# Retention attention and two expert layers on one core: order of the first loads, four sums on GpSimd, one more tile, the order of x's sums, and where h lies

## The chip, the cores and the metric

One NeuronCore of one Trainium2 chip runs the whole program in one launch. The metric is the time of the device in microseconds. The kernel before took 1574.39 us in the median of three runs (1574.02 to 1576.73).

## The reference

Inputs are float32. Three stages follow each other on the same 1536 tokens (batch 2, sequence 768) of 512 features.

```python
# 1. retention attention, 8 heads of 64, decay gamma_h = 1 - 2**(-5-h)
state = gamma * state + outer(k[t], v[t]);  y[t] = q[t] @ state / 8      # for t in 768
x = y.transpose(0, 2, 1, 3).reshape(1536, 512)
# 2. eight experts, all used for every token, Sinkhorn gates
P = exp(x @ w_gate - max);  eight times: normalise rows, then columns, times N/E
x = sum_e P[:, e:e+1] * (relu(x @ w1[e]) @ w2[e])                        # w1 512x1024, w2 1024x512
# 3. four experts with gates that come as an input (rows normalised)
out = sum_e p[:, e:e+1] * (relu(x @ w1[e]) @ w2[e])
```

## The kernel before

**Attention.** The sequence is cut into six chunks of 128 positions; with two batches that makes twelve steps s, c = s // 2 the chunk and b = s % 2 the batch. TensorE computes in step order: score(s+1) (line 893), then attend(s): the product of state and raised q (line 913, not in chunk 0), the sum of k and v into the state (line 925, not in the last chunk), and scores by v (line 931). attend(s) writes one of three PSUM banks in turn, so attend(s) from s = 3 on waits until chunk (s-3)//2 has been read out of its bank: by `x_summed` and `x_lo0`, and for a bank of batch 1 by `x_lo1` as well. VectorE masks scores (line 557). GpSimd multiplies k by a decay (line 312) and q by a rise (line 325), and waits for `y_done` before each rise. Each engine works strictly in the order in which its instructions are written.

**x.** Each float32 operand of the expert layers is held as a high and a low fp32r part. x is also needed in four sums of its quarters (names T1 to T4, tile `x_sum`), because the first product of an expert is done by seven products on half-size blocks, in place of eight. For chunk n ScalarE runs `x_high0` (line 370, batch 0), `x_high1` (line 381 copies quarter B12 into the place of T3 in `x_sum`, line 382 the high part of B22) and `sums_high` (line 386). VectorE runs `x_sums` (line 563, four subtractions; the fourth writes T3 over the copy of B12), `x_low0`, `x_low1` and `sums_low` (all line 592); for the last two chunks `sums_low` is GpSimd's (line 330). As B12 is copied into `x_sum`, `x_high1(n)` waits until `sums_low(n-1)` has read `x_sum`.

**Experts.** Each of the 12 experts is done in two halves of its 1024 hidden features, k = 0 to 23, and each of these over two blocks p of 384 positions of both batches. up(k, p) is 84 products of 384 columns (lines 1010, 1012, 1014): stationary w1_hi or w1_lo, moving x_hi or x_lo. down(k, p) is 72 products of 512 columns (lines 1031 to 1033): stationary h_hi or h_lo, moving w2_hi or w2_lo. The hidden values h are made by ScalarE and VectorE. w1 comes by one DMA of 1 MB into `w_raw`; `w1_sums` (lines 602 to 608, VectorE) makes three sums of its quarters and leaves a fourth in place; `split_w1_high` (ScalarE, lines 416 to 423) and `split_w1_low` (VectorE, line 592, parts 0 to 3) split them. w2 comes into the same `w_raw` once all four parts are done. For k = 0 all this is written into the last steps of attention: `w1_sums(0)` after VectorE's step 9, part 0 of the high halves after ScalarE's step 10, and VectorE's low parts 0 and 1 in step 11, parts 2 and 3 after `x_sums(5)`. Of up(0, 0), product 0 (12 matmuls) needs w1's low part 0; product 1 waits until ScalarE has copied product 0 out (line 467), and ScalarE has `sums_high(5)` ahead of that copy. After up(0, 0) come 40 matmuls with `wg_parts` for the gates (lines 959, 961), 384 columns, stationary `wg_parts`, moving x_hi or x_lo.

**Loads.** SP issues, in order: k_t and q_t of step 0, the mask, v and k of step 0, then q/k, v and k of step 1, and so on; from step 4 on it waits for `y_done` of step s-4 before the loads of step s. Expert w1(0) is issued after the loads of step 8. ScalarE's queue issues kdecay, rise, step, ident, w_gate and the gates of layer 3; the last two arrive in runs of 32 and 16 bytes.

**Places.** Tiles are placed in SBUF one behind the other, each from a multiple of 32 bytes. x_hi, x_lo, w1_hi, w1_lo, w2_hi and w2_lo begin at the same place modulo 512 bytes. Then come small tiles and `place`, and then, overlaid, attention's tiles or h_hi, h_lo, ups and acc: these begin 192 bytes behind that place modulo 512. `wg_parts` begins 320 bytes behind it.

Of the kernel before, what the change touches and what calls it, by code (L numbers as in the profile page):

```python
# [9 lines left out]
ALU = mybir.AluOpType  # L10
# [4 lines left out]
P = 128  # L15
BATCH, HEADS, SEQ, HD = 2, 8, 768, 64
DM = HEADS * HD
DC = DM // P
NTOK = BATCH * SEQ
NSUB = NTOK // P  # L20
# [9 lines left out]
BANK = 512  # L30
SINKHORN = 8
EPS = 1e-9
WARM = 10
GAMMA = [1.0 - 2.0 ** (-5.0 - h) for h in range(HEADS)]


# [24 lines left out]
def retention_moe_moe_kernel(nc, q_t, k_t, k, v, moe_w_gate, moe_w1, moe_w2, moe2_probs, moe2_w1, moe2_w2,  # L61
# [3 lines left out]
    with ctx:  # L65
        def sb(name, shape, dt=F32, scope=None):
            return (scope or ctx).enter_context(nc.sbuf_tensor(name, shape, dt))
# [16 lines left out]
        w2_hi = sb("w2_hi", [P, UC, DM], F32R)  # L84
        w2_lo = sb("w2_lo", [P, UC, DM], F32R)
        x_sum = sb("x_sum", [P, 4 * 2, P])
        ident = sb("ident", [P, P])
        act_warm = sb("act_warm", [P, 2])
        gate1 = sb("gate1", [P, NSUB, E1])
# [8 lines left out]
        step = sb("step", [P, DC])  # L98


        sb("place", [P, 48])

# [127 lines left out]
        @block.sync  # L232
        def _(sp):
            def load_qk(c, b):
                r = c % 2
                sp.dma_start(kt_in[r][b][:, :, :], k_t[b, c].rearrange("p (c t) -> p c t", c=DC)).then_inc(qk_in[r][b], 16)
                sp.dma_start(qt_in[r][b][:, :, :], q_t[b, c].rearrange("p (c t) -> p c t", c=DC)).then_inc(qk_in[r][b], 16)

            def load_k(c, b):
                r = c % 2  # L240
                sp.dma_start(k_in[r][b][:, :, :], k[b, c].rearrange("t (h d) -> t h d", h=HEADS)).then_inc(
                    k_in_s[r][b], 16)

            def load_v(c, b):
                r = c % 2
                sp.dma_start(v_in[r][b][:, :, :], v[b, c].rearrange("t (h d) -> t h d", h=HEADS)).then_inc(
                    v_in_s[r][b], 16)

            def load_w1(w, e, s):
                src = w[bass.ds(e, 1), :, s * UF:(s + 1) * UF].rearrange("a (c p) f -> p (a c) f", p=P)  # L250
                sp.dma_start(w1_raw, src).then_inc(w1_in, 16)

            def load_w2(w, e, s):
                src = w[bass.ds(e, 1), s * UF:(s + 1) * UF, :].rearrange("a (c p) n -> p (a c) n", p=P)
                sp.dma_start(w2_raw, src).then_inc(w2_in, 16)

            load_qk(0, 0)
            sp.dma_start(mask[:, :, :, :], c_mask.rearrange("p (r c j) -> p r c j", r=2, c=DC)).then_inc(mask_in, 16)
            load_v(0, 0)
            load_k(0, 0)  # L260
            load_qk(0, 1)
            load_v(0, 1)
            load_k(0, 1)
            for s in range(2, STEPS):
                c, b = s // BATCH, s % BATCH
                if c > 1:

                    sp.wait_ge(y_done, s - 4 + 1)
                load_qk(c, b)
                load_v(c, b)  # L270
                if c < CH - 1:
                    load_k(c, b)
                if s == 8:
                    load_w1(moe_w1, 0, 0)

            def weights(w1, w2, e, k, last=False):
                sp.wait_ge(w1_ready, 4 * k + 4)
                load_w2(w2, e, 0)
                sp.wait_ge(w2_ready, 2 * k + 2)
                load_w1(w1, e, 1)  # L280
                sp.wait_ge(w1_ready, 4 * k + 8)
                load_w2(w2, e, 1)
                if not last:
                    sp.wait_ge(w2_ready, 2 * k + 4)

            with sp.Fori(0, E1 - 1) as e:
                weights(moe_w1, moe_w2, e, 2 * e)
                load_w1(moe_w1, e + 1, 0)
            weights(moe_w1, moe_w2, E1 - 1, 2 * (E1 - 1))
            load_w1(moe2_w1, 0, 0)  # L290
            with sp.Fori(0, E2 - 1) as e:
                weights(moe2_w1, moe2_w2, e, 2 * e + 2 * E1)
                load_w1(moe2_w1, e + 1, 0)
            weights(moe2_w1, moe2_w2, E2 - 1, 2 * (E1 + E2 - 1), last=True)

            last = 2 * (E1 + E2) - 1
            stores = [(0, 3), (0, 6), (1, 1), (1, 2), (1, 3), (1, 4), (1, 5), (1, 6)]
            for p, n in stores:
                sp.wait_ge(acc_written, downs_before(last, p) + n)
                rows = [row_of(p, u) for u in (range(n - CPB, n) if p == 0 else [n - 1])]  # L300
                sp.dma_start(out_d[:, rows[0]:rows[-1] + 1, :], acc[:, rows[0]:rows[-1] + 1, :]).then_inc(stored, 16)
            sp.wait_ge(stored, 16 * len(stores))
# [3 lines left out]
        def _(pool):  # L306
# [29 lines left out]
            decay_k(0)  # L336
            decay_k(1)
            nc.gpsimd.memset(wg_parts[:, :, :].bitcast(F32), 0.0).then_inc(wg_zeroed, 1)
            for s in range(BATCH, STEPS):
                raise_q(s)  # L340
                if s < STEPS - BATCH:
                    decay_k(s)
            for n in range(CH - 2, CH):
                sums_low(n)

# [11 lines left out]
        def _(act):  # L357
            act.dma_start(kdecay[:, :, :], c_kdecay.rearrange("p (c h) -> p c h", c=CH - 1)).then_inc(kdecay_in, 16)
            act.dma_start(rise[1][:, :, :], c_rise.rearrange("p (c t) -> p c t", c=DC)).then_inc(rise_in, 16)
            act.dma_start(step[:, :], c_step).then_inc(rise_in, 16)  # L360
            act.dma_start(ident[:, :], c_ident).then_inc(ident_in, 16)
            act.dma_start(wg_raw[:, :, :], moe_w_gate.rearrange("(c p) e -> p c e", p=P)).then_inc(wg_in, 16)
            act.dma_start(gate2[:, :, :], moe2_probs.rearrange("(i p) e -> p i e", p=P)).then_inc(gate2_in, 16)

            def x_high0(n, from_acc=False):
                if from_acc:
# [6 lines left out]
            def x_high1(n, from_acc=False):  # L373
                if from_acc:
                    act.wait_ge(x2_transposed, BATCH * (n - CH) + 2)
                else:
                    act.wait_ge(y_done, BATCH * n + 2)
                if n > 0:

                    act.wait_ge(x_lot, n)  # L380
                nc.scalar.copy(x_sum[:, 4:6, :], x_bank(n, 1)[:, 0:2, :]).then_inc(x_b12, 1)
                nc.scalar.copy(x_hi[:, X_B22, :, x_at(n)], x_bank(n, 1)[:, 2:4, :]).then_inc(x_hi1, 1)

            def sums_high(n):
# [42 lines left out]
            nc.scalar.copy(act_warm[:, 1:2], act_warm[:, 0:1])  # L427
            for s in range(STEPS):
                c, b = s // BATCH, s % BATCH
                if b == 1:  # L430
                    x_high0(c)
                elif c > 0:
                    x_high1(c - 1)
                if c < CH - 1:
                    state_out(s, b)
                if b == 0 and c > 0:
                    sums_high(c - 1)
                if b == 0 and 2 <= c + 2 < CH:
                    rise_out(c + 2)
                if s == STEPS - 2:  # L440
                    split_w1_high(0, 0, first=True)
                if s == STEPS - 1:
                    split_w1_high(0, 1)
            act.wait_ge(wg_in, 16)
            act.wait_ge(wg_zeroed, 1)
            nc.scalar.copy(wg_parts[:, :, 0:E1], wg_raw[:, :, :]).then_inc(wg_hi_ready, 1)
# [95 lines left out]
        def _(dve):  # L542
# [18 lines left out]
            def x_sums(n):  # L561
                def sub(o, a, b):
                    return nc.vector.tensor_tensor(o, a, b, ALU.subtract)  # L563

                t1, t2, t3, t4 = [x_sum[:, 2 * i:2 * i + 2, :] for i in range(4)]
                y0, y1 = x_bank(n, 0), x_bank(n, 1)


                dve.wait_ge(x_b12, n + 1)

                dve.wait_ge(x_hi1, n + 1)
                then_wait(sub(t1, t3, y0[:, 0:2, :]))
                then_wait(sub(t2, y1[:, 2:4, :], t1))
                sub(t4, y0[:, 2:4, :], t2)
                sub(t3, y1[:, 2:4, :], t3).then_inc(x_summed, 1)

            def x_low0(n):
                dve.wait_ge(x_hi0, n + 1)
# [12 lines left out]
            def low(out, raw, high):  # L591
                return nc.vector.tensor_tensor(out, raw, high.bitcast(F32), ALU.subtract)  # L592

            def w1_sums(k, first=False):
                a11, a21 = w1_raw[:, 0:2, 0:2 * P], w1_raw[:, 0:2, 2 * P:4 * P]
                a12, a22 = w1_raw[:, 2:4, 0:2 * P], w1_raw[:, 2:4, 2 * P:4 * P]
                s2, s3, s4 = w1_sum[:, 0, :, :], w1_sum[:, 1, :, :], w1_sum[:, 2, :, :]
                dve.wait_ge(w1_in, 16 * k + 16)
                if not first:

                    dve.wait_ge(w1_ready, 4 * k)
                nc.vector.tensor_tensor(s3, a11, a21, ALU.subtract).then_inc(w1_summed, 1)
                dve.wait_ge(w1_summed, 4 * k + 1)
                nc.vector.tensor_tensor(a21, a21, a22, ALU.add).then_inc(w1_summed, 1)
# [40 lines left out]
            mask_scores(0)  # L645
            for s in range(STEPS):
                c, b = s // BATCH, s % BATCH
                if s < STEPS - 1:
                    mask_scores(s + 1)
                if b == 1:  # L650
                    x_low0(c)
                    if 0 < c < CH - 1:
                        sums_low(c - 1)
                elif c > 0:
                    x_sums(c - 1)
                    x_low1(c - 1)
# [476 lines left out]
```

## Time and profile before

| | |
|---|---|
| median of three runs | 1574.39 us |
| the profiled execution's own time | 1574.22 us |
| its span, first to last instruction | 1572.4 us |
| mean granted TensorE clock | 0.997 |
| TensorE busy | 1553.9 us, 99% of the span |
| VectorE, ScalarE, GpSimd busy | 884.4, 445.8, 51.4 us |

What lies around the span in the profiled execution is 1.8 us. Matmuls are pipelined: one is recorded as longer than the distance from its start to the next start, and that distance, the pitch, is what counts. Line numbers are those of the kernel before.

### The profile page before, as it was taken

The numbers are of one execution on the slowest core, as the hardware profiler recorded it, in microseconds if no ns is written. First come the engines' busy times: TensorE is split into PE (matmuls) and PEld (weight loads), VectorE is DVE, ScalarE is ACT, GpSimd is POOL, SyncE is SP. The second block draws the span as 40 slices with busy tenths as digits, with TensorE's granted clock in tenths as the row PEclk, the third lists the DMA queues.
The fourth block names the chain that finished last, engine by engine and source line by source line (L and its number), as shares of the span: only waits on it lengthen the run. The fifth ranks groups of instructions, "written<-read, shape, count | busy, mean of one in ns | idle before, by whom it ended". The sixth has DMA issues, their size and how long they took to land.

```text
span 1572.4 us, 21277 instructions
## 1 busy us (share of the span) xinstructions
PE 1553.9 (99%) x8232; PEld 1404.6 (89%) x8232; DVE 884.4 (56%) x1437; ACT 445.8 (28%) x860; POOL 51.4 (3%) x42
## 2 busy tenths in 40 slices
PE   8899999999999999999999999999999999999999
PEld 7798899889989988998899889988998899889988
DVE  6846766455555465464455554667545546545553
ACT  4422223213313222232133222333322223213321
POOL 5200000000000000000000000012000000000000
PEclk9899999999999999999999999999999999999999
DMA  9201001011010010110110100101001011011011
GB/s 325 86 3 54 26 28 54 0 54 54 1 53 27 27 53 2 51 53 0 53 38 15 53 27 28 54 0 55 27 28 54 10 45 54 0 53 53 1 42 67
DMA packets 36491, 67.28 MB, mean 43 GB/s; under 512 B 4048, under 2 KB 4176, under 8 KB 36432
## 3 DMA queue, kind: packets, MB, share of 16 engines
q1 hardware_dynamic: 33776, 66.07, 12.1%
q8 instruction: 41, 0.67, 0.2%
q10 hardware_dynamic: 2656, 0.39, 0.2%
q14 instruction: 18, 0.15, 0.0%
HBM read 63.31 MB, written 3.15 MB: 42 GB/s over the span
## 4 chain that ended last, share of the span: by engine, by line
PE 96%; DVE 2%; issue 1%; ACT 1%; DMA 1%; SPq 0%; DVEq 0%; ACTq 0%
PE bank L1032 17%; PE bank L1031 17%; PE bank L1033 17%; PE bank L1010 15%; PE bank L1014 15%; PE bank L1012 15%; DVE x_sum L563 1%; DMA qt_in<-in_q_t 1%; DVE x_lo L592 0%; PE bank L978 0%; DVE scores L557 0%; ACT rise L405 0%; PE bank L961 0%; PE bank L959 0%; ACT x_hi L370 0%
## 5 line engine op out<-in xcount | busy, mean ns | idle before, releaser
L1032 PE MATMUL bank<-w_lo,h_hi 128*128 128x512 f32 x1152 | 453.7, 394 | 0.0
L1010 PE MATMUL bank<-x_hi,w_hi 128*128 128x384 f32 x1344 | 450.6, 335 | 3.0 <-DVE w_lo L592 1.3
L1031 PE MATMUL bank<-w_hi,h_hi 128*128 128x512 f32 x1152 | 451.9, 392 | 0.0
L1014 PE MATMUL bank<-x_hi,w_lo 128*128 128x384 f32 x1344 | 450.1, 335 | 0.0
L1012 PE MATMUL bank<-x_lo,w_hi 128*128 128x384 f32 x1344 | 449.8, 335 | 0.0
L1033 PE MATMUL bank<-w_hi,h_lo 128*128 128x512 f32 x1152 | 447.3, 388 | 0.0
L756 DVE SCALAR_TENSOR_TENSOR acc<-bank,gate,acc 128x512 f32<-128x512 f32 x252 | 189.2, 751 | 379.7 <-PE bank L1033 379.7
L467 ACT COPY ups<-bank 128x384 f32<-128x384 f32 x288 | 138.7, 482 | 911.6 <-PE bank L1014 911.6
L709 DVE TENSOR_TENSOR ups<-bank,ups 128x384 f32<-128x384 f32 x288 | 155.4, 554 | 191.2 <-ACT ups L467 169.5
L1033 PEld LDWEIGHTS bank<-w_hi,h_lo 128*128 128x128 f32 x1152 | 216.3, 188 | 48.3
L1031 PEld LDWEIGHTS bank<-w_hi,h_hi 128*128 128x128 f32 x1152 | 216.2, 188 | 48.2
L1010 PEld LDWEIGHTS bank<-x_hi,w_hi 128*128 128x128 f32 x1344 | 252.8, 188 | 6.1 <-issue 2.3
L1012 PEld LDWEIGHTS bank<-x_lo,w_hi 128*128 128x128 f32 x1344 | 252.8, 188 | 1.8
L1032 PEld LDWEIGHTS bank<-w_lo,h_hi 128*128 128x128 f32 x1152 | 216.6, 188 | 41.3
L1014 PEld LDWEIGHTS bank<-x_hi,w_lo 128*128 128x128 f32 x1344 | 252.7, 188 | 0.0
L470 ACT ACTIVATE h_hi<-ups 128x384 fp32r<-128x384 f32 x288 | 148.0, 524 | 134.3 <-DVE ups L709 134.3
L714 DVE SCALAR_TENSOR_TENSOR h_lo<-ups,h_hi 128x384 fp32r<-128x384 f32 x288 | 156.2, 557 | 12.3
L592 DVE TENSOR_TENSOR w_lo<-w_raw,w_hi 128x1024 fp32r<-128x1024 f32 x96 | 114.8, 1217 | 0.0
L714 DVE SCALAR_TENSOR_TENSOR h_lo<-bank,h_hi 128x384 fp32r<-128x384 f32 x96 | 53.6, 558 | 2.2
L470 ACT ACTIVATE h_hi<-bank 128x384 fp32r<-128x384 f32 x96 | 47.3, 493 | 12.7
L330 POOL TENSOR_TENSOR x_lo<-x_sum,x_hi 128x1024 fp32r<-128x1024 f32 x8 | 20.1, 2514 | 903.8 <-ACT x_hi L386 903.8
L592 DVE TENSOR_TENSOR w_lo<-w_sum,w_hi 128x1024 fp32r<-128x1024 f32 (+1 forms) x48 | 46.3, 965 | 0.0
(76 smaller groups left out, 498.2 us busy)
## 6 DMA issues: line engine op xcount, KB each, us to landing
w_raw<-in_moe_w SPq DMA_DIRECT2D x48, 1024.0 KB, 5.1
kt_in<-in_k_t SPq DMA_DIRECT2D x12, 256.0 KB, 4.4
qt_in<-in_q_t SPq DMA_DIRECT2D x12, 256.0 KB, 5.9
v_in<-in_v SPq DMA_DIRECT2D x12, 256.0 KB, 6.0
k_in<-in_k SPq DMA_DIRECT2D x10, 256.0 KB, 6.4
out<-acc SPq DMA_DIRECT2D x2, 768.0 KB, 4.5
out<-acc SPq DMA_DIRECT2D x6, 256.0 KB, 2.0
mask<-in_c_mask SPq DMA_DIRECT2D x1, 512.0 KB, 5.7
```

The source lines that it names most:

```text
L467: nc.scalar.copy(ups[:, half, slot, :], up_psum(ON_X, half)).then_inc(copied, 1)
L470: nc.scalar.activation(h_hi[:, f, b, :], src, ACT.Relu).then_inc(h_hi_ready, 1)
L592: return nc.vector.tensor_tensor(out, raw, high.bitcast(F32), ALU.subtract)
L709: nc.vector.tensor_tensor(ups[:, half, slot, :], up_psum(kind, half), ups[:, half, slot, :], ALU.add).then_inc(summed, 1)
L714: nc.vector.scalar_tensor_tensor(h_lo[:, f, b, :], src, 0.0, h_hi[:, f, b, :].bitcast(F32), ALU.max, ALU.subtract).then_inc(h_ready, 1)
L756: nc.vector.scalar_tensor_tensor(a, y, gate[:, i, bass.ds(col, 1)], a, ALU.mult, ALU.add).then_inc(acc_written, 1)
L1010: nc.tensor.matmul(o, w1_hi[:, w, kc, fs], x_hi[:, x, kc, at], start=start and kc == 0, stop=False, skip_group_check=True)
L1012: nc.tensor.matmul(o, w1_hi[:, w, kc, fs], x_lo[:, x, kc, at], start=False, stop=False, skip_group_check=True)
L1014: last = nc.tensor.matmul(o, w1_lo[:, w, kc, fs], x_hi[:, x, kc, at], start=False, stop=kc == 1, skip_group_check=True)
L1031: nc.tensor.matmul(o, h_hi[:, f, b, rows], w2_hi[:, f, :], start=(n == 0), stop=False)
L1032: nc.tensor.matmul(o, h_hi[:, f, b, rows], w2_lo[:, f, :], start=False, stop=False)
L1033: last = nc.tensor.matmul(o, h_lo[:, f, b, rows], w2_hi[:, f, :], start=False, stop=(n == UC - 1))
```

## The change

- SP's loads come in the order of use: q and k_t of a step, then k and v of the step before. So v(0), k(0) stand behind q/k of step 1, and from step 4 on k and v of step s-1 stand behind the wait of step s. w1(0) moves from behind step 8's loads to before step 11's wait. ident and the gates of layer 3 move from ScalarE's queue to the end of SP's attention loads. w_gate and the gates of layer 3 are laid out in the partition order by the host, so that each partition is one run.
- The first w1 sums go from VectorE to GpSimd: two of them before the rise of q of step 11, two behind it.
- B12 has its own tile `b12` (1024 bytes). `x_high1(n)` then waits for `x_summed` of chunk n-1, and `x_sums(n)` waits for `x_lot`.
- VectorE's `x_sums(c-1)` is ahead of `mask_scores(s+1)` in even steps. At the end the order is low part 0, `x_low0(5)`, low parts 1, 2, 3, `x_sums(5)`, `x_low1(5)`. ScalarE's high part 0 of w1 is after `sums_high(4)` in program order as before, and its second half is behind `x_high0(5)`.
- `place` grows from 192 to 512 bytes. With b12's 1024 that moves attention's tiles and h_hi, h_lo, ups and acc by 1344 bytes: their offset modulo 512 to w2 and x goes from 192 to 0, that of `wg_parts` from 320 to 128.
- TensorE's warm-up is 8 matmuls instead of 10.

```diff
-WARM = 10
+WARM = 8
+        b12 = sb("b12", [P, 2, P])
-        sb("place", [P, 48])
+        sb("place", [P, 128])
@@ sync
+            def load_kv(c, b):
+                if c < CH - 1:
+                    load_k(c, b)
+                load_v(c, b)
             load_qk(0, 0)
...
-            load_v(0, 0)
-            load_k(0, 0)
-            load_qk(0, 1)
-            load_v(0, 1)
-            load_k(0, 1)
-            for s in range(2, STEPS):
+            for s in range(1, STEPS):
+                if s == STEPS - 1:
+                    load_w1(moe_w1, 0, 0)
                 if c > 1:
                     sp.wait_ge(y_done, s - 4 + 1)
                 load_qk(c, b)
-                load_v(c, b)
-                if c < CH - 1:
-                    load_k(c, b)
-                if s == 8:
-                    load_w1(moe_w1, 0, 0)
+                load_kv((s - 1) // BATCH, (s - 1) % BATCH)
+            load_kv(CH - 1, 1)
+            sp.dma_start(ident[:, :], c_ident).then_inc(ident_in, 16)
+            sp.dma_start(gate2[:, :, :], moe2_probs.rearrange("p (i e) -> p i e", e=E2)).then_inc(gate2_in, 16)
@@ gpsimd
+            def first_w1_sums():
+                pool.wait_ge(w1_in, 16)
+                nc.gpsimd.tensor_tensor(s3, a11, a21, ALU.subtract).then_inc(w1_summed, 1)
+                pool.wait_ge(w1_summed, 1)
+                nc.gpsimd.tensor_tensor(a21, a21, a22, ALU.add).then_inc(w1_summed, 1)
+                raise_q(STEPS - 1)
+                pool.wait_ge(w1_summed, 2)
+                nc.gpsimd.tensor_tensor(s2, a21, a11, ALU.subtract).then_inc(w1_summed, 1)
+                pool.wait_ge(w1_summed, 3)
+                nc.gpsimd.tensor_tensor(s4, a12, s2, ALU.subtract).then_inc(w1_summed, 1)
@@ scalar
-                    act.wait_ge(x_lot, n)
-                nc.scalar.copy(x_sum[:, 4:6, :], x_bank(n, 1)[:, 0:2, :]).then_inc(x_b12, 1)
+                    act.wait_ge(x_summed, n)
+                nc.scalar.copy(b12[:, :, :], x_bank(n, 1)[:, 0:2, :]).then_inc(x_b12, 1)
+                if s == STEPS - 1:
+                    split_w1_high(0, 0, first=True)
                 if b == 1:
                     x_high0(c)
...
-                if s == STEPS - 2:
-                    split_w1_high(0, 0, first=True)
-                if s == STEPS - 1:
-                    split_w1_high(0, 1)
+            split_w1_high(0, 1)
@@ vector
+                if n > 0:
+                    dve.wait_ge(x_lot, n)
                 dve.wait_ge(x_b12, n + 1)
...
-                then_wait(sub(t1, t3, y0[:, 0:2, :]))
+                then_wait(sub(t1, b12[:, :, :], y0[:, 0:2, :]))
...
-                sub(t3, y1[:, 2:4, :], t3).then_inc(x_summed, 1)
+                sub(t3, y1[:, 2:4, :], b12[:, :, :]).then_inc(x_summed, 1)
...
+                if b == 0 and c > 0:
+                    x_sums(c - 1)
                 if s < STEPS - 1:
                     mask_scores(s + 1)
-                if b == 1:
+                if b == 0 and c > 0:
+                    x_low1(c - 1)
+                elif b == 1 and c < CH - 1:
                     x_low0(c)
-                    if 0 < c < CH - 1:
+                    if c > 0:
                         sums_low(c - 1)
-                elif c > 0:
-                    x_sums(c - 1)
-                    x_low1(c - 1)
-                if s == STEPS - 3:
-                    w1_sums(0, first=True)
-                if s == STEPS - 1:
-                    split_w1_low(0, 0)
-                    split_w1_low(0, 1)
-            x_sums(CH - 1)
+            split_w1_low(0, 0)
+            x_low0(CH - 1)
+            split_w1_low(0, 1)
             split_w1_low(0, 2)
             split_w1_low(0, 3)
+            x_sums(CH - 1)
             x_low1(CH - 1)
```

## Rows read from the trace of the kernel before

**Rows 1.** The page, busy time of each engine, share of the span, instructions.
```profile
PE 1553.9 (99%) x8232; PEld 1404.6 (89%) x8232; DVE 884.4 (56%) x1437; ACT 445.8 (28%) x860; POOL 51.4 (3%) x42
```

**Rows 2.** Busy time by stretch, then granted clock (1.00 is 2.4 GHz), DMA share, GB/s.
```profile
51.20:53.60 2.40, 0.08 (x2) 0.00 (x0) 2.33 (x5) 0.00 (x0) 0.00 (x0) 0.99 0.00 0
53.60:55.60 2.00, 0.00 (x1) 0.01 (x1) 1.93 (x6) 0.03 (x1) 0.00 (x0) 0.50 0.00 0
...
60.90:63.80 2.90, 2.89 (x9) 2.90 (x10) 2.83 (x6) 0.42 (x2) 0.00 (x0) 0.50 0.00 0
...
70.00:1570.00 1500.00, 1498.15 (x7550) 1354.80 (x7548) 835.88 (x1356) 414.10 (x789) 19.23 (x15) 1.00 0.10 35
```

**Rows 3.** Timeline of TensorE in an expert layer: start, us, instruction.
```profile
707.17 0.39 PE L1031 MATMUL bank<-w_hi,h_hi 128*128 128x512 f32 x1
...
723.65 0.33 PE L1010 MATMUL bank<-x_hi,w_hi 128*128 128x384 f32 x1
...
738.23 0.39 PE L1031 MATMUL bank<-w_hi,h_hi 128*128 128x512 f32 x1
```

**Rows 4.** Timeline of TensorE around the 40 matmuls of the gates.
```profile
77.73 0.34 PE L959 MATMUL bank<-x_hi,wg_parts 128*128 128x384 f32 x1
...
84.79 0.39 PE L1031 MATMUL bank<-w_hi,h_hi 128*128 128x512 f32 x1
```

**Rows 5.** Timeline of TensorE in attention.
```profile
10.53 1.16 PE L893 MATMUL bank<-qt_in,kt_in 64*128 64x128 f32 x16 [2.83 <-DMA qt_in<-in_q_t]
...
13.55 1.16 PE L893 MATMUL bank<-qt_in,kt_in 64*128 64x128 f32 x16 [0.38 <-DMA qt_in<-in_q_t]
...
16.61 1.16 PE L893 MATMUL bank<-qt_in,kt_in 64*128 64x128 f32 x16 [0.41 <-DMA qt_in<-in_q_t]
...
20.29 1.16 PE L893 MATMUL bank<-qt_in,kt_in 64*128 64x128 f32 x16
...
37.41 1.16 PE L913 MATMUL bank<-q_up,state 128*128 128x128 f32 x8 [0.60 <-DVE x_sum L563]
...
48.00 1.16 PE L893 MATMUL bank<-qt_in,kt_in 64*128 64x128 f32 x16
...
55.60 2.08 PE L913 MATMUL bank<-q_up,state 128*128 128x128 f32 x8 [4.32 <-DVE x_sum L563]
...
60.91 0.69 PE L1010 MATMUL bank<-x_hi,w_hi 128*128 128x384 f32 x1 [1.32 <-DVE w_lo L592]
...
65.17 0.41 PE L1010 MATMUL bank<-x_hi,w_hi 128*128 128x384 f32 x1 [0.60 <-ACT ups L467]
```

**Rows 6.** Timeline of VectorE in attention and at its end.
```profile
40.86 1.74 DVE L592 TENSOR_TENSOR x_lo<-x_sum,x_hi 128x1024 fp32r<-128x1024 f32 x1
42.52 1.27 DVE L557 TENSOR_TENSOR scores<-bank,mask 128x512 f32<-128x512 f32 x2
...
48.83 1.76 DVE L602 TENSOR_TENSOR w_sum<-w_raw 128x512 f32<-128x512 f32 x1
...
59.64 1.22 DVE L592 TENSOR_TENSOR w_lo<-w_raw,w_hi 128x1024 fp32r<-128x1024 f32 x1
...
61.91 0.41 DVE L563 TENSOR_TENSOR x_sum<-x_sum,bank 128x256 f32<-128x256 f32 x1
...
63.48 0.68 DVE L592 TENSOR_TENSOR w_lo<-w_sum,w_hi 128x512 fp32r<-128x512 f32 x1
```

**Rows 7.** Timeline of ScalarE at the end of attention.
```profile
58.42 0.58 ACT L370 CAST x_hi<-bank 128x512 fp32r<-128x512 f32 x1
...
63.60 1.05 ACT L386 CAST x_hi<-x_sum 128x1024 fp32r<-128x1024 f32 x1 [2.48 <-DVE x_sum L563]
```

**Rows 8.** Timeline of GpSimd.
```profile
43.91 1.27 POOL L325 TENSOR_TENSOR q_up<-qt_in,rise 128x512 f32<-128x512 f32 x1 [0.41 <-PE bank L931]
48.26 1.78 POOL L325 TENSOR_TENSOR q_up<-qt_in,rise 128x512 f32<-128x512 f32 x1 [3.08 <-PE bank L931]
```

**Rows 9.** The page, DMA issues: size, median us to landing.
```profile
w_raw<-in_moe_w SPq DMA_DIRECT2D x48, 1024.0 KB, 5.1
```

More of the change, by code:

```diff
@@ L338, in _ @@
             nc.gpsimd.memset(wg_parts[:, :, :].bitcast(F32), 0.0).then_inc(wg_zeroed, 1)
-            for s in range(BATCH, STEPS):
+            def first_w1_sums():
+                a11, a21 = w1_raw[:, 0:2, 0:2 * P], w1_raw[:, 0:2, 2 * P:4 * P]
+                a12, a22 = w1_raw[:, 2:4, 0:2 * P], w1_raw[:, 2:4, 2 * P:4 * P]
+                s2, s3, s4 = w1_sum[:, 0, :, :], w1_sum[:, 1, :, :], w1_sum[:, 2, :, :]
+                pool.wait_ge(w1_in, 16)
[7 more added lines that the diff above has]
+                nc.gpsimd.tensor_tensor(s4, a12, s2, ALU.subtract).then_inc(w1_summed, 1)
+            for s in range(BATCH, STEPS - 1):
                 raise_q(s)
@@ L342, in _ @@
                     decay_k(s)
+            first_w1_sums()
             for n in range(CH - 2, CH):
@@ L360, in _ @@
             act.dma_start(step[:, :], c_step).then_inc(rise_in, 16)
-            act.dma_start(ident[:, :], c_ident).then_inc(ident_in, 16)
-            act.dma_start(wg_raw[:, :, :], moe_w_gate.rearrange("(c p) e -> p c e", p=P)).then_inc(wg_in, 16)
-            act.dma_start(gate2[:, :, :], moe2_probs.rearrange("(i p) e -> p i e", p=P)).then_inc(gate2_in, 16)
+            act.dma_start(wg_raw[:, :, :], moe_w_gate.rearrange("p (c e) -> p c e", e=E1)).then_inc(wg_in, 16)
             def x_high0(n, from_acc=False):
@@ L592, in low, with w1_sums @@
                 return nc.vector.tensor_tensor(out, raw, high.bitcast(F32), ALU.subtract)
-            def w1_sums(k, first=False):
+            def w1_sums(k):
                 a11, a21 = w1_raw[:, 0:2, 0:2 * P], w1_raw[:, 0:2, 2 * P:4 * P]
@@ L598, in w1_sums @@
                 dve.wait_ge(w1_in, 16 * k + 16)
-                if not first:
-                    dve.wait_ge(w1_ready, 4 * k)
+                dve.wait_ge(w1_ready, 4 * k)
                 nc.vector.tensor_tensor(s3, a11, a21, ALU.subtract).then_inc(w1_summed, 1)
@@ L1123 @@
     laid["k"], laid["v"] = _chunks_by_position(inputs["k"]), _chunks_by_position(inputs["v"])
+    laid["moe_w_gate"] = inputs["moe_w_gate"].reshape(DC, P, E1).transpose(1, 0, 2).reshape(P, DC * E1)
+    laid["moe2_domain_probs"] = inputs["moe2_domain_probs"].reshape(NSUB, P, E2).transpose(1, 0, 2).reshape(P, NSUB * E2)
     arrays, args = {}, []
```

## The prediction

> **What bounds it now.** I read the busy times first: TensorE is busy for 99% of the span, the next engine for 56% [rows 1]. From 70 to 1570 us it lacks 1.85 us of 1500, at full clock [rows 2]. So in the expert layers only the pitch of its matmuls counts, and nothing that VectorE, ScalarE or a DMA saves there. Before 66 us it is otherwise. The timeline of TensorE, with what ended each idle time, shows three kinds of loss: scores that wait for q's load (2.83, 0.38, 0.41 us), state products that wait for `x_sums` (0.60 us, three times, once per chunk; then 4.32 us), and the first expert's products behind low parts of w1 and a copy of `ups` [rows 5]. The first expert product starts at 60.91 and the second product block at 65.17; from there TensorE runs without a gap. The last state product's 4.32 us have a simple source: VectorE is in order, and it does four w1 sums from 48.83 on, the first 1.76 us, before it masks and gets to `x_sums(4)` [rows 6]. In the same stretch the granted clock is at 0.50, that is 1.2 GHz, from 53.6, some 2.4 us after TensorE went idle, to 63.8 [rows 2].
>
> I go by two sums: when does the second product block start (65.17 before), and what is the pitch of the rest.
>
> **Start of attention.** Scores 1, 2 and 3 start at 10.53, 13.55, 16.61 as their q lands [rows 5]: 3.04 us for each MB, 0.76 us for a load of 256 KB. In the new order v and k of one step (two loads) no longer stand ahead of each q, so q(3) is 1.5 us earlier, 15.1. Against it: k(0) now lands after q(1), at 10.53 - 1.5 + 0.76 = 9.8; its decay takes at most the 1.27 us of a rise of the same size [rows 8], the attend then some 1.6 us (a step without state, 3.06 less 0.41 idle less 1.1 for the scores), and k(1) is 3.0 us later: 12.8 + 1.3 + 1.6 = 15.7. That would leave 0.9. For it: 2048 runs of 16 and 32 bytes, and ident, leave the queues; each load should pass faster, by how much no row says. Bounds 0.9 and 2.4, I take 1.7. From step 4 on k and v stand behind a wait, but TensorE wants them over 2 us later than q of the next step, and a step of 1 MB takes 3.0 us of DMA against 3.68 us of TensorE [rows 5]; hidden. Two warm-up matmuls less: nothing, as score(1) waits for a load.
>
> **The pace of attention.** A step without a stall takes 3.68 us (16.61 to 20.29). From 20.29 to 48.00 are seven steps, 27.71 us, so 1.95 are stalls [rows 5]. They come from a ring: `x_sums`, `sums_high`, rise, `x_high0`, `x_low0`, `sums_low` 1.74 us, mask 1.27 us, `x_sums` [rows 6]; ScalarE's copy of B12 sits in it too, behind `sums_low`. With b12 the copy starts as soon as attend is done, and with `x_sums` ahead of the mask it ends 1.3 us earlier, which is more than 0.60. What is next is TensorE itself. The moved mask is late by 1.65 us, but its scores are wanted only 3 us later. VectorE's own work per chunk is about 6.7 us (two pairs of masks 2.5, `x_sums` 1.65, lows 0.6 + 0.35 + 1.7) of 7.36: little air, so 0 to 1.95, I take 1.95. Score(11) then starts at 48.00 - 1.7 - 1.95 = 44.35.
>
> **The end of attention**, in order. GpSimd: rise(10) ends at about 42; w1 is issued near 35.5 and takes 5.1 us [rows 9] to 8 behind the loads ahead, so at 41 to 43; two sums of 1.27 us (1.78 where VectorE reads SBUF at the same time [rows 8]), then rise(11), 43 + 2.5 + 1.3 = 46.8 at the worst guess; TensorE wants it at 47.5. Then two sums, to 49.3 at the worst. VectorE: mask(10) to 43.1, `x_low0(4)` to 43.7, `sums_low(3)` 1.74 to 45.4, `x_sums(4)` 1.65 to 47.0, mask(11) to 48.3. TensorE: scores, state product, scores by v, each about 1.05: 47.5, so attend(11) starts with no wait and ends at 49.7. ScalarE: `sums_high(4)` 1.0 to 48.1, w1 high part 0 to 49.1, part 1 to 50.0, `x_high0(5)` 0.55 to 50.5 [rows 7], then two more parts, w_gate and the two copies of `x_high1(5)` to 53. VectorE: low part 0 from 49.1, 1.13 (1.22 less the overlap of the next [rows 6]) to 50.25: product 0 starts at 50.3, was 60.91. Then `x_low0(5)` to 51.2, low part 1 to 52.3, part 2 (0.6) to 52.9, part 3 to 54.05, `x_sums(5)`. From the start of `x_sums(5)` to the second product block it was 65.17 - 61.91 = 3.26 us [rows 5, 6]; now 57.3. Gain 7.9. Parts 2 and 3 now stand ahead of `x_sums(5)`, 1.7 us on this path that the other order would not pay; the sum has them. Bounds 9 (the loads pass faster) and 5 (rise(11) or a part of w1 late by 3).
>
> **The clock.** TensorE does product 0 to 52.4 and idles to 57.3, 4.9 us, longer than the 4.4 after which it was at 1.2 GHz before [rows 2, 5]. So I expect it to start the second block at half clock. Before, nine matmuls took the 2.9 us from 60.90 to 63.80, 0.32 us each and not 0.173, and then it rose [rows 2]. If it again rises 2.9 us after work begins that costs 1.45 us; if the low stretch is 10.2 us long as before and begins 2.4 us after TensorE stops, it is 54.8 to 65.0, and 7.7 us at half speed cost 3.85; if the clock stays up, 0. I take 1.7. Net gain to here 6.2 us. After it TensorE stays the bound: w2 is issued once all w1 parts are done, 54 instead of 65.4, so everything behind moves by more than TensorE does.
>
> **The place of h.** Per block 72 matmuls of 512 columns take 723.65 - 707.17 = 16.48 us, 228.9 ns each; 84 of 384 columns take 14.58 us, 173.6 ns [rows 3]. At 2.4 GHz the columns alone are 213.3 and 160.0 ns; 15.6 and 13.6 ns lie on top. The third kind tells more: the 40 matmuls with `wg_parts`, the same moving tiles and the same 384 columns, take 77.73 to 84.79, 176.5 ns [rows 4], 2.9 more than those with w1. What differs is the stationary tile, which begins 320 bytes off modulo 512, h 192 off, w1 0. So stationary and moving operand at one place modulo 512 look 2.0 to 3 ns cheaper. With h at 0 I expect 160.0's surcharge, 13.3 to 13.6: 226.8 ns. There are 48 x 72 = 3456 such matmuls: 2.0 to 2.3 ns are 6.9 to 7.9 us; I take 7.4. Bounds 0 (the extra comes with the width) and 10 (2.9 ns).
> The Trainium skill, "TensorE: Matmul & The Clock Gate", Part 2, speaks against this: TensorE has two independent SBUF read ports, so loading the next weights takes nothing from the running matmul. By that rule the place of h would not matter and the whole would come to rival 1. The trace bears it out only in part: the loads are hidden, but the pitch does depend on the stationary tile, 176.5 against 173.6 ns.
>
> Nothing else in the layers counts: the logits' 40 matmuls may move by 0.1 us; VectorE's new wait on `x_lot` at the change of layers asks for nothing that ScalarE's copy did not wait for.
>
> **Sum.** 1574.22 (span 1572.4 and 1.8 around it; the median is 1574.39, 0.01% off) - 6.2 - 7.4 = 1560.6.
>
> **Rivals.**
> 1. The place does nothing; the 2 ns belong to 512 columns. For: only one other width is in the trace, and the logits' matmuls reuse weights in pairs, not threes. Against: their 176.5 ns. Time 1574.2 - 6.2 = 1568.0. Chance 0.2.
> 2. Place as forecast, but attention gives half: GpSimd's sums hold rise(11), since w1 is now issued some 6 us later, or shared reading of SBUF makes VectorE's operations 1.7 instead of 1.2 us, four of them on the path: 3 us lost. For: 48.83's 1.76 us beside the rise's 1.78 [rows 6, 8]. Against: rise(11) has 0.7 us to spare. Time 1563.8. Chance 0.15.
> 3. The other side: two reads that begin at one place modulo 512 hinder each other, and the pitch of the 3456 rises. It outweighs 6.2 us from 1.8 ns per matmul on; at 3 ns, as much as the gates' matmuls are above w1's, it costs 10.4: 1578.4. Against: w1 and x lie so and have the least surcharge. Chance 0.03.
> 4. The loads do not do what they say (the order in the queue is not the order of landing): then 1.7 goes, 1562.3; within the forecast's range.
>
> The forecast with rival 4 has 0.62. Its own range is 1558.3 to 1563. The range for 8 in 10 runs from 1557.8 to 1568.6, to take in rival 1. A measurement tells 0.2%, 3.1 us, from no change. Faster by more: 0.95; same 0.02 (attention gives under half and the place nothing); slower 0.03.
>
> **What would show it.** Score(11) near 44.4 and no wait of the state products for `x_sums`; product 0 near 50.3; the second block near 57.3, with matmuls of 0.32 us for some 3 us; 72 matmuls of a down block in 16.3 us; `wg_parts` still near 176 ns. A pitch of 228.9 ns would be rival 1; a second block after 59.5 rival 2. It is wrong if TensorE has new idle time after 70 us.

## The result and the profile after

The changed kernel takes 1565.34 us in the median of four runs, the one before 1575.09 us: a ratio of 0.9939, 95% interval 0.9922 to 0.9957. It is faster by 0.6%. The forecast was 1560.6 us, range 1557.8 to 1568.6. Each kernel's trace is of one execution. In the profiled executions the span went from 1572.4 to 1563.1 us, 9.3 us, where 13.6 were forecast.

TensorE's timeline in attention, start and us as in [rows 5] (scores 3, the last scores, the last state product, products 0 and 1 of the first up block):
```profile
14.82 1.16 PE L907 MATMUL bank<-qt_in,kt_in 64*128 64x128 f32 x16
...
44.91 1.16 PE L907 MATMUL bank<-qt_in,kt_in 64*128 64x128 f32 x16 [0.65 <-DMA qt_in<-in_q_t]
...
48.67 1.13 PE L927 MATMUL bank<-q_up,state 128*128 128x128 f32 x8 [0.49 <-POOL q_up L327]
...
50.88 0.45 PE L1024 MATMUL bank<-x_hi,w_hi 128*128 128x384 f32 x1
...
60.31 0.66 PE L1024 MATMUL bank<-x_hi,w_hi 128*128 128x384 f32 x1 [7.07 <-ACT ups L481]
```
The four waits for `x_sums` are gone. The last state product now waits 0.49 us for GpSimd's rise of q, where the forecast had no wait. Product 0 starts 10.0 us earlier than in [rows 5], but product 1 only 4.9 us earlier: TensorE now stands idle for 7.07 us between them.

How early all this starts differs from execution to execution, so single traces are best compared from scores 3 on. In the eight traces of this section and the next whose loads are in the changed order and whose clock is at full speed from 8.6 us on, scores 3 start at 14.00 to 15.19 us. In e4, b3 and e5, described below, the clock was at half for 3.4 to 6.8 us between 8.9 and 15.7, and scores 3 start at 16.31, 16.68 and 17.63. The kernel before has 16.61, and 18.49 in e1, whose clock was at half as well. From scores 3 to product 1 it is 48.56 us before (48.82 in e1) and 45.49 in the changed kernel (44.68 to 45.50 in e2 to e5 and b3).

Busy time by stretch, columns as in [rows 2]: the granted clock is at half after that stall too.
```profile
53.10:56.30 3.20, 0.14 (x1) 0.00 (x0) 3.20 (x3) 1.13 (x4) 1.21 (x1) 1.00 0.00 0
56.30:60.30 4.00, 0.00 (x0) 0.02 (x1) 3.49 (x11) 1.56 (x3) 0.43 (x1) 0.50 0.45 120
60.30:63.10 2.80, 2.79 (x9) 2.80 (x10) 0.66 (x2) 0.73 (x2) 1.92 (x1) 0.50 0.52 203
64.00:1560.00 1496.00, 1494.86 (x7564) 1356.81 (x7562) 833.93 (x1354) 414.50 (x790) 19.17 (x15) 1.00 0.10 35
```
Nine matmuls took 2.8 us there, 1.3 us more than at full clock. This too differs between executions with the same stall: the half clock lasted 2.7 us behind product 1 here, 3.6 in b3 and 5.9 in e4.

An expert's down block and up block, and the 40 matmuls of the gates, as in [rows 3, 4]:
```profile
74.18 0.34 PE L973 MATMUL bank<-x_hi,wg_parts 128*128 128x384 f32 x1
...
81.22 0.39 PE L1045 MATMUL bank<-w_hi,h_hi 128*128 128x512 f32 x1
...
701.20 0.39 PE L1045 MATMUL bank<-w_hi,h_hi 128*128 128x512 f32 x1
...
717.56 0.33 PE L1024 MATMUL bank<-x_hi,w_hi 128*128 128x384 f32 x1
...
732.15 0.39 PE L1045 MATMUL bank<-w_hi,h_hi 128*128 128x512 f32 x1
```
The down block takes 16.36 us, 227.2 ns per matmul; before it was 16.48. The up block is 14.59, as before; the gates' 7.04 (7.06). The other down blocks differ by as much or nearly, and 48 by 0.12 are 5.8 us. So the span's 9.3 us are 4.9 of an earlier product 1, less 1.3 for the clock that was already back before, and 5.8 of pitch: 9.4.

Why product 1 is late: the ends of GpSimd, VectorE and ScalarE, in this order, one view each.
```profile
43.66 2.26 POOL L346 TENSOR_TENSOR w_sum<-w_raw 128x512 f32<-128x512 f32 x1 [1.62 <-DMA w_raw<-in_moe_w]
...
49.83 2.15 POOL L353 TENSOR_TENSOR w_sum<-w_raw,w_sum 128x512 f32<-128x512 f32 x1
51.94 2.38 POOL L332 TENSOR_TENSOR x_lo<-x_sum,x_hi 128x1024 fp32r<-128x1024 f32 x1
```
```profile
48.80 2.02 DVE L608 TENSOR_TENSOR w_lo<-w_raw,w_hi 128x1024 fp32r<-128x1024 f32 x1 [0.53 <-ACT w_hi L431]
51.34 0.69 DVE L608 TENSOR_TENSOR x_lo<-bank,x_hi 128x512 fp32r<-128x512 f32 x1 [0.51 <-ACT x_hi L385]
51.95 4.04 DVE L608 TENSOR_TENSOR w_lo<-w_sum,w_hi 128x1024 fp32r<-128x1024 f32 x2
...
57.05 0.41 DVE L577 TENSOR_TENSOR x_sum<-b,bank 128x256 f32<-128x256 f32 x1
```
```profile
49.78 1.05 ACT L434 CAST w_hi<-w_sum 128x1024 fp32r<-128x1024 f32 x1 [1.01 <-POOL w_sum L351]
...
58.74 1.05 ACT L401 CAST x_hi<-x_sum 128x1024 fp32r<-128x1024 f32 x1 [4.51 <-DVE x_sum L577]
```
VectorE's low part 0 takes 2.02 us beside GpSimd's sum, parts 1 and 2 together 4.04 beside GpSimd's `sums_low(4)`; the one in [rows 6] took 1.22 alone. ScalarE waits a further microsecond for a sum of GpSimd. `x_sums(5)` starts at 57.05; the distance from there to product 1 is 3.26 us, as before.

### The profile page after: what moved, and what is told of

Same layout as the page of the kernel before. It is cut to its first block, busy times and chain, and to the rows that moved or that the text cites. A ratio compares the mean times of both kernels' runs of the same rounds, so it can differ in the third digit from the quotient of the medians.

```text
span 1563.1 us, 21269 instructions
## 1 busy us (share of the span) xinstructions
PE 1546.8 (99%) x8228; PEld 1403.1 (90%) x8228; DVE 881.2 (56%) x1433; ACT 446.4 (29%) x860; POOL 56.5 (4%) x46
## 4 chain that ended last, share of the span: by engine, by line
PE 97%; DMA 1%; DVE 1%; POOL 0%; SPq 0%; ACT 0%; issue 0%; POOLq 0%
PE bank L1047 17%; PE bank L1046 17%; PE bank L1045 17%; PE bank L1024 15%; PE bank L1028 15%; PE bank L1026 15%; DMA w_raw<-in_moe_w 1%; PE bank L907 0%; DMA k_in<-in_k 0%; PE bank L945 0%; PE bank L927 0%; PE bank L992 0%; PE bank L939 0%; DVE w_lo L608 0%; PE bank L973 0%; PE bank L975 0%
## 5 line engine op out<-in xcount | busy, mean ns | idle before, releaser
L1046 PE MATMUL bank<-w_lo,h_hi 128*128 128x512 f32 x1152 | 449.0, 390 | 0.0
L728 DVE SCALAR_TENSOR_TENSOR h_lo<-bank,h_hi 128x384 fp32r<-128x384 f32 x96 | 53.5, 557 | 2.3
```

The source lines that it names most:

```text
L728: nc.vector.scalar_tensor_tensor(h_lo[:, f, b, :], src, 0.0, h_hi[:, f, b, :].bitcast(F32), ALU.max, ALU.subtract).then_inc(h_ready, 1)
L1046: nc.tensor.matmul(o, h_hi[:, f, b, rows], w2_lo[:, f, :], start=False, stop=False)
```

## Experiments

Each was run beside the kernel before. e3, e4, e5, a3, b1, b2 and b3 ran once each: their traces are read, and a time given for one of them has no interval.

**Place alone, and the rest alone.** e1 is the kernel before, e2 the changed kernel, each with one number changed.
```diff
-        sb("place", [P, 48])      # e1
+        sb("place", [P, 128])
-        sb("place", [P, 128])     # e2
+        sb("place", [P, 48])
```


> The kernel before with place grown from 192 to 512 bytes and nothing else: h, ups and acc go to offset 0 modulo 512. My theory: the pitch of the down matmuls falls from 228.9 to the 227.3 ns seen in the changed kernel, 3456 of them save 5.8 us; attention is untouched (second product block at 65.2). Time 0.9963 of before. Rival (the place does nothing, the pitch fell through something else of the change): 228.9 ns, ratio 1.000.

> The changed kernel with place back at 192 bytes, h at offset 192. My theory: pitch back to 228.9 ns, attention as in the changed kernel (second product block at 60.3, then some 3 us at half clock), so 0.9978 of before: 3.4 us. Rival (the gain lies in attention): at or under 0.995.

e1: ratio 0.9962 (0.9949 to 0.9974), e2: 0.9975 (0.9965 to 0.9984). Their product is 0.9937, the change's 0.9939: the two parts add up, 6.0 and 3.9 us, with 2 us of interval to either side of the first and 1.5 of the second. e1's product 1 started at 67.31 and not at 65.2 as expected, because its first loads came late (scores 3 at 18.49) and the clock fell in them; e2's at 59.87, as expected. Start of a down block and of what follows it, e1 and then e2:
```profile
708.43 0.39 PE L1031 MATMUL bank<-w_hi,h_hi 128*128 128x512 f32 x1
...
724.79 0.33 PE L1010 MATMUL bank<-x_hi,w_hi 128*128 128x384 f32 x1
```
```profile
703.46 0.39 PE L1045 MATMUL bank<-w_hi,h_hi 128*128 128x512 f32 x1
...
719.94 0.33 PE L1024 MATMUL bank<-x_hi,w_hi 128*128 128x384 f32 x1
```
16.36 and 16.48 us. The place sets the pitch, alone and in full; rival 1 is out.

**Which distance.** h begins 256 bytes (e3) or 128 bytes (e5) behind w2's place modulo 512, and in b3 all tiles move by 64 bytes together.
```diff
-        sb("place", [P, 128])
+        sb("place", [P, 64])      # e3; [P, 32] in e5
+        sb("shift", [P, 16])      # b3, ahead of x_hi
```


> The changed kernel with place of 256 bytes: h at offset 256, half way. If any offset but 0 costs the same, 228.9 ns. If it grows with the distance modulo 512, more than 228.9, up to 229.5 to 230 (the gates' weights at 320 cost 2.9 ns, h at 192 2.3). If only a step of the offset matters to writes, 227.

> The changed kernel with place of 128 bytes: h begins 128 bytes behind w2's place modulo 512. At 0 and at 256 the down matmuls took 227.3 ns, at 192 228.9. Theory A (any multiple of 128 is good, 64 off is not): 227.3 ns. Theory B (only multiples of 256 are good): 228.9 ns or so.

> The changed kernel with 64 unused bytes ahead of all tiles: everything moves by 64 bytes, h and w2 (and x and w1) keep their distance of 0. Theory A (the distance of stationary and moving tile modulo 256 counts): 227.3 ns per down matmul, 173.4 per up matmul. Theory B (each tile's own place counts): down above 228.9, up at 176 to 177, as the gates' matmuls at an odd 64; that is 10 us or more of span.

The same two rows of e3, then e5 (ahead of them in both the gates' matmuls), then b3:
```profile
74.61 0.34 PE L973 MATMUL bank<-x_hi,wg_parts 128*128 128x384 f32 x1
...
81.65 0.39 PE L1045 MATMUL bank<-w_hi,h_hi 128*128 128x512 f32 x1
...
701.63 0.39 PE L1045 MATMUL bank<-w_hi,h_hi 128*128 128x512 f32 x1
...
717.99 0.33 PE L1024 MATMUL bank<-x_hi,w_hi 128*128 128x384 f32 x1
```
```profile
77.49 0.33 PE L973 MATMUL bank<-x_hi,wg_parts 128*128 128x384 f32 x1
...
84.42 0.39 PE L1045 MATMUL bank<-w_hi,h_hi 128*128 128x512 f32 x1
...
711.84 0.39 PE L1045 MATMUL bank<-w_hi,h_hi 128*128 128x512 f32 x1
...
728.57 0.34 PE L1024 MATMUL bank<-x_hi,w_hi 128*128 128x384 f32 x1
```
```profile
703.45 0.39 PE L1046 MATMUL bank<-w_hi,h_hi 128*128 128x512 f32 x1
...
719.81 0.33 PE L1025 MATMUL bank<-x_hi,w_hi 128*128 128x384 f32 x1
```
16.36, 16.73 and 16.36 us: 227.2 ns at distance 0 and 256, 228.9 at 192, 232.4 at 128; the run with 128 took 1585.9 us, more than before the change. In e5 theory A is out, and theory B (only multiples of 256 are good) is right in kind but not in size: 128 is the worst distance seen, not a middling one. With everything moved by 64 the pitch stays, so it is the distance of the tiles that counts and not where each begins. The gates' matmuls agree: 7.06 us for 40 at distance 320, 7.04 at 128 and, in e3, at 384, and 6.93 in e5, where `wg_parts` lies at 256. Modulo 512 in the change's words is thus modulo 256 in these runs. As x, w1 and w2 begin at one place in all of them, the distance to the moving tile and that to the other tiles were not told apart.

**The first nine matmuls.** In the changed kernel the first nine of a down block take 2.08 us, the last nine 2.04; the tenth of the block above is
```profile
703.28 0.39 PE L1045 MATMUL bank<-w_hi,h_hi 128*128 128x512 f32 x1
```
e4 moves ups and acc back to 192 and leaves h.
```diff
+            sb("pad", [P, 48], F32, moe)
             ups = sb("ups", [P, 2, 3, BLK], F32, moe)
```


> The changed kernel with 192 unused bytes between h_lo and ups: h stays at 0, ups and acc go back to 192. In the changed kernel the first nine matmuls of a down block take 231 ns and not 226.7, while VectorE and ScalarE write the last h. Theory A: it is their traffic on ups at offset 0; then all 72 take 226.7, the mean 226.7, and 2 us go. Theory B: it is the traffic on h_hi and h_lo itself; then the nine stay at 231 and the mean at 227.3.

```profile
704.16 0.39 PE L1046 MATMUL bank<-w_hi,h_hi 128*128 128x512 f32 x1
...
720.52 0.33 PE L1025 MATMUL bank<-x_hi,w_hi 128*128 128x384 f32 x1
```
The down block stays at 16.36 us, with the first nine slow, so it is not where ups lies. That leaves theory B, the traffic on h itself, by exclusion only.

**ScalarE's order.** a1 asks whether product 1 needs what it waits for.
```diff
             def unit(k, p, x2=None, sums=None):
-                if sums is not None:
-                    sums_high(sums)
                 for half in range(2):
                     hidden_copy(k, p, 0, half, U_P1)
                 for half in range(2):
                     hidden_copy(k, p, 1, half, U_U2)
+                if sums is not None:
+                    sums_high(sums)
```


> The changed kernel, with ScalarE's sums_high(5) moved behind its copies of products 0 and 1 of up(0, 0). My theory: the 7.1 us before the second product block come only from ScalarE's order, since the copy needs nothing but product 0; so the block starts right behind product 0, near 53.1 and not 60.3, and the clock stays at 2.4 GHz. Some of it comes back as a wait at product 3 or 6, since x_sums(5) ends at 58.7 and w2 is split by VectorE only at 66: TensorE would want the first hidden sum at 63.5, so 2 to 3 us are given back. Net 5 to 6.5 us less than the changed kernel: ratio 0.990. Rival (the block really waits for x or w1 parts): starts after 57, ratio 0.993 or above.

```profile
55.23 0.69 PE L1024 MATMUL bank<-x_hi,w_hi 128*128 128x384 f32 x1 [2.21 <-DVE w_lo L608]
```
and by stretch:
```profile
53.00:58.60 5.60, 3.39 (x12) 3.37 (x12) 5.53 (x8) 2.27 (x7) 1.09 (x1) 0.70 0.11 12
58.60:64.00 5.40, 5.40 (x33) 5.40 (x32) 2.60 (x8) 2.38 (x4) 2.40 (x1) 1.00 0.51 182
```
Product 1 starts at 55.23 and not at 60.31; ratio 0.9903 (0.9886 to 0.992), 1559.37 us. I had expected it at 53.1, right behind product 0, and 2 to 3 us given back at products 3 or 6. Neither came: VectorE's low part 1 is the next wait, still held up by GpSimd, and nothing was given back. The clock did not stay up either: after the 2.21 us it is 0.70 in the mean to 58.6. The theory that ScalarE's order was the wait is shown. That the time came out as expected is luck, as the two misses, of 2.1 us later and of 2 to 3 us not given back, cancel.

**w1 earlier.** a2 tests that the late sums of w1 cost the 3 us.
```diff
-                if s == STEPS - 1:
+                if s == 9:
                     load_w1(moe_w1, 0, 0)
```


> The changed kernel with w1(0) issued ahead of step 9's loads, as before the change, and not ahead of step 11's. My theory of the 3 us that product block 2 starts later than forecast (60.3 for 57.3): w1 lands at 43.6, so GpSimd's sums run at 43.7 to 52 beside VectorE's low parts, which take 2.02 and 4.04 us in place of 1.2 and 1.9. Landed by 40, GpSimd starts them at 42.1, and the second block starts at 57.5 to 58.5. Rival (GpSimd's sum of x, 51.9 to 54.3, is what slows VectorE, and it moves with the rest): 59.5 to 60.3. TensorE's 0.65 us wait for the last q goes in both.

TensorE, GpSimd and VectorE of a2, one view each:
```profile
59.01 0.66 PE L1024 MATMUL bank<-x_hi,w_hi 128*128 128x384 f32 x1 [5.84 <-ACT ups L481]
```
```profile
49.62 3.39 POOL L332 TENSOR_TENSOR x_lo<-x_sum,x_hi 128x1024 fp32r<-128x1024 f32 x1
```
```profile
51.26 3.43 DVE L608 TENSOR_TENSOR w_lo<-w_sum,w_hi 128x1024 fp32r<-128x1024 f32 x2
```
Product 1 starts 1.3 us earlier, between my theory (57.5 to 58.5) and the rival (59.5 to 60.3), but 0.8 of that is the early start of this execution: scores 3 begin at 14.00. From there it is 45.01 us, and e2 and e3, with w1 where the change has it, have 44.68 and 44.87. So the earlier w1 brings nothing that can be told from the spread, and nothing of the time (0.9946, 0.993 to 0.9963, beside the change's 0.9939). The GpSimd work moved, and `sums_low(4)` still lies on VectorE's parts, 3.39 us for 2.38. The collision moves with the work. The half clock lasted 5.7 us behind product 1 here, 3.0 more than in the changed kernel's trace, so from product 1 to the end it is 1.4 us longer.

**The clock.** a3 fills the stall with work whose result nobody reads.
```diff
+                    if first and n == 1:
+                        for i in range(36):
+                            nc.tensor.matmul(bank[4][:, 0:BLK], w1_hi[:, W_A11, 0, 0:P], x_hi[:, X_B11, 0, 0:BLK],
+                                             start=True, stop=True, skip_group_check=True)
```


> The changed kernel with 36 matmuls of 384 columns, whose result nobody reads, behind product 0 of up(0, 0), to keep TensorE at work in its 7.1 us stall: 6.2 us of them. Theory: the clock stays at 2.4 GHz; the second block starts at 60.3 as before but runs at 0.173 us per matmul, and the span is 1.4 us shorter. Rival (the fillers delay the block or the clock falls all the same): no gain, or longer.

Busy time by stretch, a3:
```profile
53.10:60.00 6.90, 5.94 (x35) 5.62 (x34) 5.67 (x13) 1.81 (x3) 1.34 (x2) 1.00 0.36 105
60.00:63.00 3.00, 3.00 (x19) 3.00 (x18) 1.50 (x3) 0.48 (x1) 1.23 (x1) 1.00 0.28 108
```
and its product 1:
```profile
60.81 0.33 PE L1028 MATMUL bank<-x_hi,w_hi 128*128 128x384 f32 x1
```
The clock stays at 2.4 GHz where it was at 1.2. Product 1 starts 0.5 us later than in the changed kernel, but from there to the end it is 1501.4 us and not 1502.8. Idleness of TensorE set the clock back, worth 1.4 us in that trace; the span, 1562.2 us, is 0.9 less.

**Loads and masks.** b1 puts SP's order of q, k and v back, b2 VectorE's order of mask and `x_sums`.
```diff
+            load_v(0, 0)          # b1, and so on as before the change
...
-                load_kv((s - 1) // BATCH, (s - 1) % BATCH)
+                load_v(c, b)
...
-                if b == 0 and c > 0:      # b2: the two are exchanged
-                    x_sums(c - 1)
                 if s < STEPS - 1:
                     mask_scores(s + 1)
+                if b == 0 and c > 0:
+                    x_sums(c - 1)
```


> The changed kernel with SP's loads of q, k and v in the order of the kernel before (w1, ident, the gates of layer 3 and the layouts as changed). Forecast by the landings: scores 3, at 14.8 in the changed kernel, starts near 16.3, and every later step 1.3 to 1.5 us later; TensorE pays it in full, since attention runs without stalls from there. Rival (VectorE's or GpSimd's chain has that much air): second product block still near 60.3.

> The changed kernel with VectorE's mask_scores(s+1) ahead of x_sums(c-1) again; b12 stays. Theory A (the tile of its own is what ended the 0.6 us stalls): no wait of a state product for x_sums before the last, steps of 3.67 us. Theory B (the order did it): waits of 0.3 to 0.6 us per chunk come back. For the last state product x_sums(4) is later by a mask, 1.2 us, so some 0.7 us of wait.

TensorE of b1, then of b2:
```profile
14.70 1.16 PE L913 MATMUL bank<-qt_in,kt_in 64*128 64x128 f32 x16
...
59.86 0.66 PE L1030 MATMUL bank<-x_hi,w_hi 128*128 128x384 f32 x1 [5.84 <-ACT ups L487]
```
```profile
35.08 1.16 PE L927 MATMUL bank<-q_up,state 128*128 128x128 f32 x8 [0.59 <-DVE x_sum L577]
...
50.08 1.16 PE L927 MATMUL bank<-q_up,state 128*128 128x128 f32 x8 [1.14 <-DVE x_sum L577]
...
61.27 0.66 PE L1024 MATMUL bank<-x_hi,w_hi 128*128 128x384 f32 x1 [3.57 <-ACT ups L481]
```
b1: scores 3 start at 14.70, not later at all, and product 1 at 59.86. 14.70 lies among the eight traces with the new order (14.00 to 15.19), so the order of q, k and v brings nothing that this trace shows; my expectation of 1.3 to 1.5 us was wrong. What then makes scores 3 1.8 us earlier than in [rows 5] is among what b1 keeps: ident and the gates of layer 3 off ScalarE's queue, w_gate and those gates in long runs, and two warm-up matmuls less. That was not split further. b2: two waits of 0.6 us come back (35.08, and another at 43.09), with 1.14 at the last, so the tile b12 alone does not end them; whether the order would without b12 was not run.

**The next version.** b4 joins four edits.
```diff
-                if s == STEPS - 1:        # and sums_high(5) later, as in a1
+                if s == 9:
...
-            for n in range(CH - 2, CH):   # GpSimd
-                sums_low(n)
+            sums_low(CH - 1)
...
             split_w1_low(0, 1)            # VectorE
+            sums_low(CH - 2)
             split_w1_low(0, 2)
...
-            split_w2(0, first=True)
             hidden(0, 0)
+            split_w2(0, first=True)
```


> The changed kernel with four edits: sums_high(5) behind the copies of products 0 and 1 (5.1 us earlier second block in its own run), w1 issued ahead of step 9's loads (1.3 us), sums_low(4) on VectorE between low parts 1 and 2 in place of GpSimd, where it held VectorE's low parts up (3.43 us for two that take 2.3), and VectorE's hidden(0, 0) ahead of its split of the first w2, which would keep product 6 waiting. Theory: second block at 52.5 to 53.5, clock at 2.4 GHz throughout, span 1555.5, ratio to before 0.988 to 0.989. Rival (the next bound is VectorE's hidden sums or w2): waits of TensorE of 1 to 3 us between 60 and 80, ratio 0.990 as with the first edit alone.

TensorE's product 0 and its following stretches in b4, then VectorE's low part 1:
```profile
52.05 0.44 PE L1024 MATMUL bank<-x_hi,w_hi 128*128 128x384 f32 x1 [1.32 <-DVE w_lo L607]
...
54.25 0.33 PE L1024 MATMUL bank<-x_hi,w_hi 128*128 128x384 f32 x1
```
```profile
50.00:60.00 10.00, 8.68 (x60) 8.43 (x57) 9.27 (x16) 6.73 (x13) 1.57 (x2) 1.00 0.17 59
60.00:100.00 40.00, 40.00 (x215) 36.85 (x214) 18.84 (x32) 9.07 (x20) 2.45 (x2) 1.00 0.11 39
```
```profile
52.52 1.21 DVE L607 TENSOR_TENSOR w_lo<-w_sum,w_hi 128x1024 fp32r<-128x1024 f32 x1
```
With `sums_low(4)` off GpSimd, low parts 1 and 2 take 1.21 and 0.68 us and not 4.04 together: that sum was what held them up. Product 1 follows product 0 without a gap at 54.25 (expected 52.5 to 53.5; product 0 itself came at 52.05), the clock stays up, and TensorE has no idle time from 60 to 100 us. The ratio to before is 0.9877 (0.986 to 0.9893), 1557.19 us; span 1555.7. It beats both kernels.

## Why the prediction was right, and where it was off

- *What bounds it*: right. The gain is the start of product 1, the clock behind it and the pitch, and nothing else: these come to 9.4 us, and the span gave 9.3.
- *The range*: 1565.34 us lies outside 1558.3 to 1563, which the prediction calls the forecast's own range. It lies inside the range for 8 in 10 because that was stretched for rival 1, which e1 and e2 exclude. In this the hit is luck; rival 2, at 1563.8, was the nearest (1560.6 and the 3 us it names make 1563.6).
- *Start of attention*: 1.7 us forecast, 1.8 measured (16.61 to 14.82; by the eight traces 1.4 to 2.6), but the agreement is luck. I derived 1.5 from the order of q, k and v; b1 shows nothing of it. What carries it is in what b1 keeps and stays open. The small runs, for which I had no price, are one candidate: in the trace before, the layer-3 gates landed only 16.1 us after their issue.
- *Pace*: right. From scores 4 on there is no stall but the last load of q, 0.65 us, behind w1, which the change issues ahead of it: an item I had left out. It is not in every execution: e2 and a3, with the same order, have none. The last scores started at 44.91, forecast 44.35.
- *End of attention*: product 0 at 50.88, forecast 50.3. Product 1 at 60.31, forecast 57.3: this is the step that failed, by 3.0 us. From scores 3 to product 1 the change gains 3.1 us where 6.2 were forecast. It is rival 2's mechanism and size: rise(11) ended at 48.5 for 46.8 and cost 0.49 us of TensorE, and reading SBUF together cost the rest. I added VectorE's low parts at 1.13 and 0.6 us although [rows 8] and 48.83 of [rows 6] showed 1.78 and 1.76 when both engines read SBUF, and the change puts GpSimd's last two w1 sums and `sums_low(4)` beside them. Low part 0 took 2.02 us for 1.22, parts 1 and 2 took 4.04; b4, without `sums_low(4)` on GpSimd, shows the cause of the latter. The Trainium skill, "SBUF — State Buffer", "Who interferes with whom", says that a VectorE instruction with two SBUF inputs contends with a GpSimd instruction that reads SBUF, and that the contention is an exclusive lock. The trace agrees: parts 1 and 2 (1.21 and 0.68 us in b4) and the sum beside them (2.38) add up to 4.27, against 4.04.
- *I missed the cheapest step*: the copy that product 1 waited for needed nothing of `x_sums(5)`. a1 moved one call and gained 5.1 us of product 1.
- *The clock*: forecast a loss of 1.7, measured 1.3; a3 shows the cause. How long the half clock lasts differs between executions, so the nearness is worth little.
- *The place*: forecast 7.4, measured 5.8 in the trace and 6.0 in time (e1). The mechanism was right, the term was mis-sized: 63 of 72 matmuls do go at the pitch I expected, 226.7, but the first nine take 231, which I had not foreseen; the last h is being written beside them. And the reason I gave, one place modulo 512, is too narrow: 256 does as well.
- Sum: 3.0 of product 1, 1.6 of pitch, less 0.4 of clock are 4.2 of the 4.3 us between forecast and span.

## What to carry to other kernels

- When a matmul stream is the bound, compare its pitch between stages of the same width; a few ns more in one of them can be the distance of its tiles in SBUF. Here 320 more unused bytes were worth 0.4%, and a distance of 128 bytes has down blocks 0.37 us longer than a distance of 0: 17.8 us in 48, or 1.1%.
- Work given to GpSimd was not free here while VectorE read both operands from SBUF. Put it where VectorE reads PSUM, or leave it on VectorE, as b4 does with `sums_low(4)`.
- Before reading a difference of a microsecond from two traces, look at how much unchanged stages differ between executions. Scores 3 started within 14.00 to 17.63 us in kernels with the same code up to there.
- At the hand-over of two stages look at each in-order engine's queue for an instruction that stands ahead of the awaited one and that nobody wants yet.

## What the runs showed of the hardware

- The pitch of 512-column fp32r matmuls depends on the distance between stationary and moving tile: 227.2 ns at 0 and 256 bytes, 228.9 at 192, 232.4 at 128; moving all tiles by 64 bytes changes nothing. For 384 columns 173.3 ns at 256 (6.93 us for 40), 176.0 at 128 and 384, and 176.5 at 320.
- The first nine matmuls of an aligned block take 231 ns, beside VectorE's and ScalarE's last writes of h; at distance 192 they did not differ from the rest. Why is open.
- The clock fell in or right behind idle times of TensorE of 4.3 us [rows 5], 7.07 us, and in a1 2.21 us, and in e1 once more at 67.6, behind idle times of 1.66 and 1.91 us before products 0 and 1. It stayed up in a3 and b4, whose idle times there were 1.0 to 1.4 us. With the same 7.1 us of idle time it stayed at half for 2.7, 3.6, 3.8 and 5.9 us of the work behind (the changed kernel, b3, e5, e4).
- VectorE's operations with two operands in SBUF and GpSimd's lengthen each other: a low part of 1.22 us took 2.02 beside a w1 sum, and the sums of 1.28 took 2.15 and 2.26. `x_low0(5)`, whose one operand is in PSUM, took 0.69 us in that stretch, as in the kernel before.
